# Attention and two gated layers on one core: output weights split earlier, transposes first, keys summed by two engines, another load order, two products in the drain

## The chip, the core and the metric

The kernel is one program on one core of a Trainium2 chip. TensorE multiplies and transposes into PSUM; VectorE (DVE), ScalarE (ACT) and GpSimd (POOL) work on what lies in SBUF, the first two on PSUM as well; SyncE (SP) issues every transfer between HBM and SBUF. Each engine runs its own list of instructions in order, and semaphores tie the lists together. The metric is the device time of one launch in microseconds (us). The kernel before took a median of 912.01 us over three runs, from 910.64 to 913.53.

## The reference

The input is attention with pooled keys and values, and two feed-forward layers behind it, all in float32:

```python
k_p = k.reshape(B, H, Sp, pool, D).mean(axis=3)          # B 4, H 8, S 576, D 64, pool 8
v_p = v.reshape(B, H, Sp, pool, D).mean(axis=3)          # Sp = 72
scores = scale * np.matmul(q, k_p.transpose(0, 1, 3, 2))
attn = softmax(scores)                                   # along the 72 keys
x = np.matmul(attn, v_p)                                 # then [2304 tokens, 512]
xn = x / rms(x) * rms_g                                  # layer 1: 512 -> 1536 -> 512
x = (silu(xn @ w_gate) * (xn @ w_val)) @ w_out
h = x @ w_in                                             # layer 2: 512 -> 2048 -> 512
out = silu(h) @ w_out2
```

`softmax` and `rms` stand for the written-out forms.

## The kernel before, in words

**Attention.** The 2304 tokens are 18 tiles of 128. For a batch element the 8 x 72 pooled rows of keys (values) are 576 rows of 512 numbers, loaded as five chunks of 128 rows (the last one has 64) into one of two `kv` slots. Summing eight neighbours is done for key batches 0 and 1 by DVE in one reduction per chunk group (`sum_keys`, L846), and otherwise by POOL in three halving additions (L505, L509, L513). DVE spreads the sums by masks into `kpm` (L855, keys) or `vb` (L871, values); TensorE transposes `kpm` (L1112) and ACT copies it to `kT` (L774).

A tile then goes through: transpose of q (L1122), scores (L1133), maximum and subtraction on DVE (`shift`, L881 and L886), exponential on ACT (L596), transpose of the weights (`prT`, L1144) and its copy on ACT (L779), the product with `vb` (L1161, "pv"), division on DVE (`divide`, L901 to L908), squares on ACT (L604), the reciprocal root on POOL (`ms` L564, `rstd` L569), its application on ACT (L609), transpose to features (L1174) and the scaled copy on DVE (L894). A hand-written list `order` sets how the steps of different tiles are interleaved; each engine walks the same list. Step s holds the scores of tile s, the `prT` of tile s-1, the q transpose of tile s+1, the x transpose of tile s-4 and the pv of tile s-1. While this runs, DVE makes the four sums of the first token block (`token_part` 0 to 3, L930 to L938) and its low halves (L942), from the x steps 6 to 14 on.

**Feed-forward.** The matrices are multiplied by a seven-product form of the 2 x 2 block product (`PRODUCTS`), in each of which a number is a high half plus a low half, with three matmuls per product of halves (L1227 to L1229). A unit is the seven products of 256 columns of an up-projection for 768 tokens: G (gate) and V (value) in layer 1. A "down" is the output projection that follows a pair of units (L1266 to L1268, 48 matmuls). Units run 0 (G), 1 (V), 2 (G), down 0, 3 (V), 4 (G), down 1 and so on.

**Weights.** Every raw weight block has to be loaded (`load_raw`), for a unit summed on POOL (`weight_sums`, L528 to L533, four instructions), rounded to high halves on ACT (`weight_high`, L629 to L634 or L622) and subtracted to low halves on POOL (`ring_low`, L540 to L546, four instructions, or `out_low`, L552 and L553 for an output block). POOL works through the list `made` in order: unit weights r0, r1, r2, output weights o0, r3, then r4, r5, o1 and on. r0 and the sums of r1 are made inside attention, between the `rstd` instructions; the rest begins when the last `rstd` is out. In ACT's list o0 stands behind the four high halves of the gated values (L704) of units 0 and 1, and r3 stands directly behind o0 and ahead of the silu of unit 2 (L686).

**Transfers.** SP issues all loads in one list: key and value batches, q tiles (`load_q(n)` waits until the q transpose of tile n-2 is done, since there are two buffers), raw weights. The loads of raw_a and raw_b (512 KB each) stand behind batch 1 of the keys, and batch 2 of keys and values stands behind q tile 4.

**First instructions.** POOL makes the identity and the masks; TensorE waits for all of them (`const_made`). DVE clears four pads and makes the mask tables, then waits for the first three chunks of keys.

Of the kernel before, what the change touches and what calls it, by code (L numbers as in the profile page):

```python
# [20 lines left out]
def ffn_kernel(nc, q, k, v, w_gate, w_val, w_out, rms_g, w2_in, w2_out, out):  # L21
# [13 lines left out]
    HB = H // 2  # L35
    H0 = [c * P // SP for c in range(RC)]
# [3 lines left out]
    FRONT = (3, 2)  # L40
# [32 lines left out]
    order = order[:order.index(("pv", NT - 1)) + 1] + [("x", NT - 3), ("unit", 0), ("x", NT - 1)]  # L73

# [58 lines left out]
    made = [("r", 0), ("r", 1), ("r", 2), ("o", 0), ("r", 3)]  # L133
# [64 lines left out]
    with ctx:  # L198
# [107 lines left out]
        s_const, s_kmask, s_pad = sem("const_made"), sem("kmask_made"), sem("pad_cleared")  # L306
# [3 lines left out]
        s_front = [sem("k0_front_loaded"), sem("v0_front_loaded")]  # L310
        s_frontsum = [sem("k0_front_summed"), sem("v0_front_summed")]
# [25 lines left out]
        def _(sp):  # L337
            def load_kv(b, kind):
                if b >= 2:
                    sp.wait_ge((s_ksum, s_vsum)[kind], b - 1)  # L340
                rows_v, done, dst = (k_rows, v_rows)[kind], (s_k, s_v)[kind][b % 2], KV[b % 2][kind]
                full, c0 = (RC - 1) * P, 0
                if b == 0:
                    c0 = FRONT[kind]
                    sp.dma_start(dst[:, 0:c0, :], rows_v[b, 0:c0 * P, :].rearrange("(c p) x -> p c x", p=P))\
                      .then_inc(s_front[kind], 16)
# [68 lines left out]
            load_q(0)  # L415
            load_kv(0, 1)
            load_q(1)
# [58 lines left out]
        def _(pool):  # L476
            level = [0]

            def step(ins):
# [7 lines left out]
            step(pool.affine_select(out=ident[:, :], in_=ident[:, :], compare_op=ALU.not_equal, fill=1.0,  # L487
                                    base=0, pattern=[[-1, P]], channel_multiplier=1))
# [71 lines left out]
            for n in range(NT):  # L560
# [9 lines left out]
                if n == 1:  # L570
                    weight_sums(0)
# [12 lines left out]
            ring_low(1)  # L584
            for i in range(2, len(made)):
# [7 lines left out]
        def _(act):  # L593
# [126 lines left out]
            def act_unit(x):  # L720
# [41 lines left out]
            for what, n in order:  # L762
# [20 lines left out]
                elif what == "pv":  # L783
# [38 lines left out]
        def _(dve):  # L822
            for i in range(2):
                for kind in range(2):
                    dve.memset(KV[i][kind][LAST:P, RC - 1, :], 0.0).then_inc(s_pad, 1)
            dve.wait_ge(s_const, 1)
            dve.tensor_scalar(vmask8[:, :, :], vmask[:, :, :], 1.0 / POOL, None, ALU.mult).then_inc(s_kmask, 1)
            for c in range(RC):
                e = H0[c] % 2
                dve.tensor_tensor(kmask[:, c, e:e + 1], vmask[:, c, 0:1], vmask[:, c, 2:3], ALU.add)\  # L830
                   .then_inc(s_kmask, 1)
                dve.tensor_copy(kmask[:, c, 1 - e:2 - e], vmask[:, c, 1:2]).then_inc(s_kmask, 1)
            for i in range(2):
                dve.tensor_copy(vb[i][:, :, :, D], vmask[:, :, :]).then_inc(s_kmask, 1)
            dve.wait_ge(s_kmask, 2 * RC + 3)
            dve.wait_ge(s_pad, 4)

            def sum_keys(b, part):
                lo, hi = (0, FRONT[0]) if part == 0 else (FRONT[0], RC)
                if b == 0 and part == 0:  # L840
                    dve.wait_ge(s_front[0], 16)
                else:
                    dve.wait_ge(s_k[b], 32)
                if b:
                    dve.wait_ge(s_kpm, b)
                ins = dve.tensor_reduce(kvp[:, 0, lo:hi, :],  # L846
                                        KV[b][0][:, lo:hi, :].rearrange("p c (r d) -> p c d r", r=POOL),
                                        AX.X, ALU.add)
                if part:
                    ins.then_inc(s_ksum, 1)  # L850
# [492 lines left out]
```

## Time and profile before

| what | us |
|---|---|
| median of three runs | 912.01 |
| the profiled execution, on its own | 909.02 |
| its span in the trace | 907.3 |
| TensorE busy in the span | 881.8 (97%) |
| TensorE busy, first 20 us | 8.62 |
| TensorE busy, 20 to 160 us | 129.2 of 140 |
| TensorE busy, 160 to 300 us | 140.00 of 140 |
| DVE busy | 519.0 (57%) |
| ACT busy | 341.4 (38%) |
| POOL busy | 252.2 (28%) |
| transfers | 191.67 MB, mean 211 GB/s |

The span runs from the first to the last instruction on the core; 909.02 is that same execution timed from outside, 1.7 us more, and 3.0 us under the median of the three plain runs. Busy time of TensorE is modelled from pipelined matmuls, so that a full slice need not be a slice at peak. Attention takes about the first 110 us, the feed-forward layers the rest.

### The profile page before, as it was taken

How to read it: one execution, taken by the hardware profiler on the slowest of the kernel's cores; microseconds unless marked ns; L12 is line 12 of the kernel's file. 1: busy time of each engine (PE TensorE's matmuls, PEld its weight loads, DVE VectorE, ACT ScalarE, POOL GpSimd, SP SyncE). 2: the span in 40 equal slices, each digit the busy share in tenths (PEclk: the TensorE clock that was granted, in tenths of full speed). 3: DMA queues.
4: the chain of work that ended last, by engine and by line, in shares of the span. 5: the costliest groups of instructions: out<-in, count | busy, mean ns of one | idle time of the engine just before them, and what ended most of it. 6: DMA issues, size and time to landing. Idle time of an engine off the chain costs nothing.

```text
span 907.3 us, 12808 instructions
## 1 busy us (share of the span) xinstructions
PE 881.8 (97%) x4902; PEld 831.6 (92%) x4902; DVE 519.0 (57%) x865; ACT 341.4 (38%) x668; POOL 252.2 (28%) x266
## 2 busy tenths in 40 slices
PE   4998998999999999999999999999999999999998
PEld 4887898999999999998989999999999898989897
DVE  7789863877655666666554445666554554343433
ACT  2566844444222232354554222322233332322322
POOL 2776378988200000637775000000000000000000
PEclk9999999999999999999999999999999999999999
DMA  9844256777875555257669666555544545475321
GB/s 273 224 126 122 104 203 236 280 279 278 336 283 204 209 209 209 79 223 277 244 255 390 240 233 248 204 205 204 207 183 181 201 174 209 174 277 175 128 90 73
DMA packets 55725, 191.67 MB, mean 211 GB/s; under 512 B 21872, under 2 KB 32112, under 8 KB 42608
## 3 DMA queue, kind: packets, MB, share of 16 engines
q1 hardware_dynamic: 55664, 190.85, 58.3%
q8 instruction: 39, 0.64, 0.3%
q14 instruction: 22, 0.18, 0.1%
HBM read 134.74 MB, written 56.10 MB: 210 GB/s over the span
## 4 chain that ended last, share of the span: by engine, by line
PE 85%; POOL 6%; issue 4%; DVE 2%; DMA 2%; ACT 1%; SPq 1%; POOLq 0%; ACTq 0%; DVEq 0%
PE ps L1227 15%; PE ps L1229 15%; PE ps L1228 15%; PE ps L1293 7%; PE ps L1294 7%; PE ps L1292 7%; PE ps L1268 5%; PE ps L1266 5%; PE ps L1267 5%; PE ps L1161 1%; PE ps L1133 1%; DMA qs<-in_q 1%; POOL wr L545 1%; POOL wr L546 1%; POOL rstd L569 1%
## 5 line engine op out<-in xcount | busy, mean ns | idle before, releaser
L1227 PE MATMUL ps<-xh,wr 128*128 128x384 f32 x840 | 281.8, 335 | 2.0 <-DVE qt L958 1.4
L1229 PE MATMUL ps<-xh,wr 128*128 128x384 f32 x840 | 281.2, 335 | 0.0
L1228 PE MATMUL ps<-xl,wr 128*128 128x384 f32 x840 | 280.9, 334 | 0.0
L1227 PEld LDWEIGHTS ps<-xh,wr 128*128 128x128 f32 x840 | 157.7, 188 | 4.5 <-DVE qt L958 3.0
L1228 PEld LDWEIGHTS ps<-xl,wr 128*128 128x128 f32 x840 | 157.7, 188 | 0.9
L1229 PEld LDWEIGHTS ps<-xh,wr 128*128 128x128 f32 x840 | 157.7, 188 | 0.0
L1294 PE MATMUL ps<-wo,al 128*128 128x512 f32 x288 | 112.5, 391 | 0.0
L1293 PE MATMUL ps<-wo,ah 128*128 128x512 f32 x288 | 112.4, 390 | 0.0
L1292 PE MATMUL ps<-wo,ah 128*128 128x512 f32 x288 | 112.0, 389 | 0.0
L1008 DVE TENSOR_TENSOR xacc<-ps,xacc 128x384 f32<-128x384 f32 (+1 forms) x102 | 62.5, 613 | 81.2 <-PE ps L1268 50.4
L1266 PE MATMUL ps<-ah,wo 128*128 128x384 f32 x288 | 97.2, 338 | 2.8 <-ACT qt L686 2.5
L704 ACT ACTIVATE ah<-qt 128x384 fp32r<-128x384 f32 x96 | 44.9, 517 | 139.2 <-PE ps L1294 126.2
L1268 PE MATMUL ps<-ah,wo 128*128 128x384 f32 x288 | 96.8, 336 | 0.0
L1267 PE MATMUL ps<-al,wo 128*128 128x384 f32 x288 | 96.8, 336 | 0.0
L995 DVE TENSOR_TENSOR al<-qt,ah 128x384 fp32r<-128x384 f32 x96 | 51.9, 583 | 73.3 <-ACT ah L704 73.3
L689 ACT ACTIVATE qt<-qt 128x384 f32<-128x384 f32 x126 | 65.5, 524 | 56.5 <-DVE qt L977 55.7
L977 DVE TENSOR_TENSOR qt<-ps,qt 128x384 f32<-128x384 f32 x84 | 46.2, 555 | 34.4 <-PE ps L1229 33.9
L1294 PEld LDWEIGHTS ps<-wo,al 128*128 128x128 f32 x288 | 54.0, 188 | 11.3
L1293 PEld LDWEIGHTS ps<-wo,ah 128*128 128x128 f32 x288 | 54.0, 188 | 10.8
L1292 PEld LDWEIGHTS ps<-wo,ah 128*128 128x128 f32 x288 | 54.1, 188 | 10.7
L704 ACT ACTIVATE ah<-vt 128x384 fp32r<-128x384 f32 x72 | 35.6, 520 | 66.3 <-DVE vt L988 66.3
L1266 PEld LDWEIGHTS ps<-ah,wo 128*128 128x128 f32 x288 | 54.6, 190 | 3.5 <-ACT qt L686 2.8
(128 smaller groups left out, 1152.6 us busy)
## 6 DMA issues: line engine op xcount, KB each, us to landing
wr<-ring_home SPq DMA_DIRECT2D x40, 1792.0 KB, 7.3
ring_home<-wr SPq DMA_DIRECT2D x20, 1792.0 KB, 8.1
wo<-out_home SPq DMA_DIRECT2D x28, 1024.0 KB, 4.8
out_home<-wo SPq DMA_DIRECT2D x14, 1024.0 KB, 9.5
raw_c<-in_moe_w_out SPq DMA_DIRECT2D x13, 512.0 KB, 7.1
qs<-in_q SPq DMA_DIRECT2D x16, 256.0 KB, 4.0
kv<-in_k SPq DMA_DIRECT2D x3, 1024.0 KB, 7.1
kv<-in_v SPq DMA_DIRECT2D x3, 1024.0 KB, 8.6
```

What stands on the lines that cost most here:

```text
L689: act.activation(qt[:, c, :], qt[:, c, :], ACT.Silu).then_inc(s_silu, 1)
L704: act.activation(ah[:, c, :], hidden(n)[:, c, :], ACT.Copy).then_inc(s_hi, 1)
L1008: dve.tensor_tensor(part, done, part, ALU.add).then_inc(s_rot, 1)
L1227: pe.matmul(out_ps, w_hi, x_hi, start=first and c == 0, stop=False, skip_group_check=True)
L1228: pe.matmul(out_ps, w_hi, x_lo, start=False, stop=False, skip_group_check=True)
L1229: ins = pe.matmul(out_ps, w_lo, x_hi, start=False, stop=c == 1, skip_group_check=True)
L1266: pe.matmul(out_ps, w_hi, h_hi, start=(rot or ends[0]) and c == 0, stop=False, skip_group_check=True)
L1267: pe.matmul(out_ps, w_hi, h_lo, start=False, stop=False, skip_group_check=True)
L1268: ins = pe.matmul(out_ps, w_lo, h_hi, start=False, stop=(rot or ends[1]) and c == 1, skip_group_check=True)
L1292: pe.matmul(out_ps, h_hi, w_hi, start=(rot or ends[0]) and c == 0, stop=False, skip_group_check=True)
L1293: pe.matmul(out_ps, h_hi, w_lo, start=False, stop=False, skip_group_check=True)
L1294: ins = pe.matmul(out_ps, h_lo, w_hi, start=False, stop=(rot or ends[1]) and c == 1, skip_group_check=True)
```

## The change

It has six parts.

1. **Start.** TensorE waits for the identity alone and runs 36 transposes of it into a PSUM bank that nobody reads (`WARM`). The mask tables and three of the four pads move from DVE to POOL. Key batch 0 is loaded as chunk 0, chunks 1 and 2, chunk 3 and the half chunk 4 (`KPARTS`); DVE sums chunks 0 to 3 in three reductions, POOL sums chunk 4.
2. **Load order.** q tile 1 goes ahead of value batch 0, key batch 2 ahead of q tile 4, and the two raw weight blocks behind q tile 5.
3. **Token sums.** `token_part` 0 to 3 move from x steps (6, 6, 7, 7) to (5, 6, 6, 8).
4. **Weights inside attention.** The sums of r0 move from POOL's n = 1 to n = 5, its low halves from 10 to 11; its high halves on ACT move one step later. The output block o0 stands second in `made`: high halves on ACT at pv 13, low halves on POOL at n = 14.
5. **Drain.** The first two products of unit 0 are issued ahead of pv 16 and pv 17.
6. **Waits.** The first unit of a phase waits for the low half of each product's operand, not for all seven.

```diff
-    FRONT = (3, 2)
+    KPARTS, VFRONT = [(0, 1), (1, 3), (3, RC - 1)], 2
+    for i in range(2):
+        order.insert(order.index(("pv", NT - 2 + i)), ("first", i))
-    made = [("r", 0), ("r", 1), ("r", 2), ("o", 0), ("r", 3)]
+    made = [("r", 0), ("o", 0), ("r", 1), ("r", 2), ("r", 3)]
...
             load_kv(0, 0)
             load_q(0)
+            load_q(1)
             load_kv(0, 1)
-            load_q(1)
             load_q(2)
             load_kv(1, 0)
...
-            load_raw(0)
-            load_raw(1)
             load_q(3)
             load_kv(1, 1)
+            load_kv(2, 0)
             for n in range(4, NT):
                 load_q(n)
-                if n in (4, 8):
-                    load_kv(n // 4 + 1, 0)
-                    load_kv(n // 4 + 1, 1)
+                if n == 4:
+                    load_kv(2, 1)
+                if n == 5:
+                    load_raw(made_at["r", 0])
+                    load_raw(made_at["r", 1])
...
-                if n == 1:
-                    weight_sums(0)
-                if n == 10:
+                if n == 5:
+                    weight_sums(0)
+                if n == 11:
                     ring_low(0)
                 if n == 12:
-                    weight_sums(1)
+                    weight_sums(made_at["r", 1])
+                if n == 14:
+                    out_low(made_at["o", 0])
...
-                    if n in (7, 8, 9):
-                        weight_high(0, (n - 7,))
+                    if n in (8, 9, 10):
+                        weight_high(0, (n - 8,))
+                    if n == 13:
+                        weight_high(made_at["o", 0])
...
-                    for i in {6: (0, 1), 7: (2, 3)}.get(n, (n - 4,) if 8 <= n < 15 else ()):
+                    for i in {5: (0,), 6: (1, 2), 7: (), 8: (3, 4)}.get(n, (n - 4,) if 9 <= n < 15 else ()):
...
-                if u == first_unit[ph]:
-                    pe.wait_ge(s_xlo, NF * (ph + 1))
-                for i, (bank, fw, fx, first) in enumerate(PRODUCTS):
+                for i, (bank, fw, fx, first) in list(enumerate(PRODUCTS))[begin:end]:
+                    if u == first_unit[ph]:
+                        pe.wait_ge(s_xlo, NF * ph + fx + 1)
...
-            pe.wait_ge(s_const, 1)
+            pe.wait_ge(s_ident, 1)
+            for _ in range(WARM):
+                pe.transpose(ps[:, 7, 0:P], ident[:, :], ident[:, :])
```

SP's list before, from the raw weights of the first units to the q tiles behind value batch 2:

```order
L370 DMA raw_a<-in_moe_w_gate 128x4x256
L370 DMA raw_b<-in_moe_w_val 128x4x256
L356 DMA qs<-in_q 128x8x64 [waits qT_made]
L347 DMA kv<-in_v 128x4x512
L349 DMA kv<-in_v 64x512
L356 DMA qs<-in_q 64x8x64 [waits qT_made]
L356 DMA qs<-in_q 64x8x64
L347 DMA kv<-in_k 128x4x512 [waits k_summed]
L349 DMA kv<-in_k 64x512
L347 DMA kv<-in_v 128x4x512 [waits v_summed]
L349 DMA kv<-in_v 64x512
L356 DMA qs<-in_q 128x8x64 [waits qT_made] x4
```

The same stretch of SP's list after the change; the two 64-row loads are q tile 4, and the q row behind value batch 2 is q tile 5:

```order
L365 DMA qs<-in_q 128x8x64 [waits qT_made]
L356 DMA kv<-in_v 128x4x512
L358 DMA kv<-in_v 64x512
L356 DMA kv<-in_k 128x4x512 [waits k0_part_summed,k_summed]
L358 DMA kv<-in_k 64x512
L365 DMA qs<-in_q 64x8x64 [waits qT_made]
L365 DMA qs<-in_q 64x8x64
L356 DMA kv<-in_v 128x4x512 [waits v0_front_summed,v_summed]
L358 DMA kv<-in_v 64x512
L365 DMA qs<-in_q 128x8x64 [waits qT_made]
L379 DMA raw_a<-in_moe_w_gate 128x4x256
L379 DMA raw_b<-in_moe_w_val 128x4x256
```

The raw weights left their place ahead of q tile 3 and stand behind q tile 5, and key batch 2 is ahead of q tile 4.

POOL's list before, at the end of r2 and the start of r3:

```order
L545 TENSOR_TENSOR wr<-wt,wr 128x512 [waits w_hi_made]
L546 TENSOR_TENSOR wr<-wt,wr 128x512
L552 TENSOR_TENSOR wo<-raw_f,wo 128x512 [waits w_hi_made]
L553 TENSOR_TENSOR wo<-raw_f,wo 128x512
L528 TENSOR_TENSOR wt<-raw_g 128x256 [waits w_raw_loaded6,ring_stored0,product_made]
```

The same place after the change:

```order
L572 TENSOR_TENSOR wr<-wt,wr 128x512 [waits w_hi_made]
L573 TENSOR_TENSOR wr<-wt,wr 128x512
L555 TENSOR_TENSOR wt<-raw_g 128x256 [waits w_raw_loaded6,ring_stored0,product_made]
L556 TENSOR_TENSOR wt<-raw_g 128x256
L558 TENSOR_TENSOR wt<-wt,raw_g 128x256 [waits w_sum_made]
```

The two instructions of o0 are gone from between r2 and r3; they stand between two `rstd` pairs inside attention.

TensorE's list after the change, from the x transpose of tile 14 into pv 17; before, the six matmul rows with `wr` were not there:

```order
L1191 MATMUL ps<-ident,xs 128x128 [waits xT_copied,xn_made]
L1191 MATMUL ps<-ident,xs 128x128 x3
L1244 MATMUL ps<-xh,wr 128x384 [waits shifted,x_lo_made,w_lo_made]
L1245 MATMUL ps<-xl,wr 128x384
L1246 MATMUL ps<-xh,wr 128x384
L1244 MATMUL ps<-xh,wr 128x384
L1245 MATMUL ps<-xl,wr 128x384
L1246 MATMUL ps<-xh,wr 128x384
L1178 MATMUL ps<-vb,prT 128x130 [waits x_made,v_blocks_made,prT_copied]
```

One product, six matmuls, stands between the transposes of a tile and the pv that waits for ACT's copy.

## Rows read from the trace of the kernel before

**Rows 1.** Stretches: length, busy us and count of each engine, clock, DMA.
```profile
0.00:20.00 20.00, 8.62 (x34) 7.34 (x35) 13.56 (x26) 3.81 (x5) 5.66 (x22) 1.00 0.95 268
120.00:140.00 20.00, 17.09 (x95) 16.13 (x94) 12.08 (x19) 7.61 (x14) 13.11 (x14) 1.00 0.75 283
140.00:150.00 10.00, 9.74 (x47) 9.74 (x48) 2.20 (x4) 3.82 (x8) 9.12 (x11) 0.83 0.44 185
...
160.00:300.00 140.00, 140.00 (x807) 139.71 (x806) 91.09 (x148) 51.27 (x96) 65.01 (x58) 1.00 0.73 281
```

**Rows 2.** Timeline of the start: start, us, engine, what, [idle before].
```profile
12.01 1.81 POOL L505 TENSOR_TENSOR kv<-kv 128x768 f32<-128x768 f32 x1 [8.79 <-DMA kv<-in_v]
12.99 2.26 PE L1133 MATMUL ps<-kT,qT 128*128 128x144 f32 x8 [0.83 <-ACT kT L774]
...
14.98 0.59 POOL L513 TENSOR_TENSOR kvp<-kv 128x192 f32<-128x192 f32 x1
...
16.76 1.15 DVE L871 TENSOR_TENSOR vb<-kvp,vmask 128x960 f32<-128x960 f32 x1
...
19.28 0.76 DVE L881 TENSOR_REDUCE mx<-ps 128x8 f32<-128x576 f32 x1 [1.38 <-PE ps L1133]
...
27.58 1.25 PE L1133 MATMUL ps<-kT,qT 128*128 128x144 f32 x8
...
29.21 0.60 PE L1122 MATMUL ps<-ident,qs 128*128 128x128 f32 x4
...
35.70 0.66 PE L1122 MATMUL ps<-ident,qs 128*128 128x128 f32 x4 [0.34 <-DMA qs<-in_q]
```

**Rows 3.** The chain that ended last, 20 to 40 us: start, us, what.
```profile
23.11 0.52 SPq L349
...
26.00 9.65 DMA qs<-in_q
```

**Rows 4.** Transfers issued from 23.1 to 23.6 us: size, us to landing.
```profile
kv<-in_k SPq DMA_DIRECT2D x1, 128.0 KB, 8.0
```

**Rows 5.** Timeline of the middle of attention, DVE, TensorE and POOL.
```profile
74.47 0.94 DVE L935 TENSOR_TENSOR xt<-xacc,xt 128x768 f32<-128x768 f32 x1
...
77.59 1.93 PE L1161 MATMUL ps<-vb,prT 128*128 128x130 f32 x12 [1.28 <-DVE xs L908]
...
80.98 1.71 PE L1133 MATMUL ps<-kT,qT 128*64 128x144 f32 x16 [1.46 <-issue]
...
84.91 2.09 DVE L942 TENSOR_TENSOR xl<-xacc,xh 128x768 fp32r<-128x768 f32 x1
...
86.13 2.00 POOL L546 TENSOR_TENSOR wr<-wt,wr 128x512 fp32r<-128x512 f32 x1
```

**Rows 6.** Timeline from the drain to unit 4, all engines.
```profile
104.17 1.97 PE L1161 MATMUL ps<-vb,prT 128*128 128x130 f32 x12 [0.41 <-ACT prT L780]
...
108.04 1.96 PE L1161 MATMUL ps<-vb,prT 128*128 128x130 f32 x12 [0.77 <-ACT prT L780]
...
113.66 1.28 POOL L540 TENSOR_TENSOR wr<-raw_b,wr 128x512 fp32r<-128x512 f32 x1
...
118.53 0.42 PE L1227 MATMUL ps<-xh,wr 128*128 128x384 f32 x1
...
126.40 0.44 PE L1227 MATMUL ps<-xh,wr 128*128 128x384 f32 x1 [0.33 <-POOL wr L546]
...
131.47 1.29 POOL L552 TENSOR_TENSOR wo<-raw_f,wo 128x512 fp32r<-128x512 f32 x1 [5.13 <-ACT wo L622]
...
137.95 0.63 ACT L629 ACTIVATE wr<-raw_g 128x512 fp32r<-128x512 f32 x1 [6.55 <-POOL wt L533]
...
140.26 0.69 PE L1266 MATMUL ps<-ah,wo 128*128 128x384 f32 x1 [2.46 <-ACT qt L686]
...
143.62 0.37 PE L1267 MATMUL ps<-al,wo 128*128 128x384 f32 x1
...
159.15 0.44 PE L1227 MATMUL ps<-xh,wr 128*128 128x384 f32 x1 [1.44 <-DVE qt L958]
```

More of the change, by code:

```diff
@@ L35, in ffn_kernel @@
     HB = H // 2
+    WARM = 36
     H0 = [c * P // SP for c in range(RC)]
@@ L309, in ffn_kernel @@
         s_v = [sem(f"v_loaded{i}") for i in range(2)]
-        s_front = [sem("k0_front_loaded"), sem("v0_front_loaded")]
-        s_frontsum = [sem("k0_front_summed"), sem("v0_front_summed")]
+        s_kpart = [sem(f"k0_part_loaded{i}") for i in range(2)]
+        s_vfront, s_kpartsum, s_vfrontsum = sem("v0_front_loaded"), sem("k0_part_summed"), sem("v0_front_summed")
         s_kpmfront = sem("k0_front_masked")
@@ L486, in _ @@
             step(pool.memset(vmask[:, :, :], 1.0))
-            step(pool.affine_select(out=ident[:, :], in_=ident[:, :], compare_op=ALU.not_equal, fill=1.0,
-                                    base=0, pattern=[[-1, P]], channel_multiplier=1))
+            pool.affine_select(out=ident[:, :], in_=ident[:, :], compare_op=ALU.not_equal, fill=1.0,
+                               base=0, pattern=[[-1, P]], channel_multiplier=1).then_inc(s_ident, 1)
             for c in range(RC):
@@ L499, in _ @@
             last.then_inc(s_const, 1)
+            pool.wait_ge(s_const, 1)
+            pool.tensor_scalar(vmask8[:, :, :], vmask[:, :, :], 1.0 / POOL, None, ALU.mult).then_inc(s_kmask, 1)
+            for c in range(RC):
+                e = H0[c] % 2
+                pool.tensor_tensor(kmask[:, c, e:e + 1], vmask[:, c, 0:1], vmask[:, c, 2:3], ALU.add)\
+                    .then_inc(s_kmask, 1)
+                pool.tensor_copy(kmask[:, c, 1 - e:2 - e], vmask[:, c, 1:2]).then_inc(s_kmask, 1)
+            for i in range(2):
+                pool.tensor_copy(vb[i][:, :, :, D], vmask[:, :, :]).then_inc(s_kmask, 1)
+            pool.wait_ge(s_kmask, 2 * RC + 3)
+            for i, kind in ((0, 1), (1, 0), (1, 1)):
+                pool.memset(KV[i][kind][LAST:P, RC - 1, :], 0.0).then_inc(s_pad, 1)
             def pool_pairs(b, kind, lo, hi):
                 t, n = KV[b % 2][kind], POOL * D // 2
-                pool.wait_ge(s_pad, 4)
+                pool.wait_ge(s_pad, 3)
+                if (b, kind) == (0, 0):
+                    pool.wait_ge(s_pad0, 1)
                 pool.wait_ge((s_k, s_v)[kind][b % 2], 32 * (b // 2 + 1))
@@ L578, in _ @@
                             pool_rest(b, kind, 0)
-                if n == 10:
+                if n == 5:
+                    weight_sums(0)
+                if n == 11:
                     ring_low(0)
                 if n == 12:
-                    weight_sums(1)
-            ring_low(1)
-            for i in range(2, len(made)):
+                    weight_sums(made_at["r", 1])
+                if n == 14:
+                    out_low(made_at["o", 0])
+            ring_low(made_at["r", 1])
+            for i in range(3, len(made)):
                 if made[i][0] == "r":
@@ L822, in _, with sum_keys @@
         def _(dve):
[L823 to L850, printed above, removed]
-                elif b == 0:
-                    ins.then_inc(s_frontsum[0], 1)
+            def sum_keys(b, lo, hi):
+                return dve.tensor_reduce(kvp[:, 0, lo:hi, :],
+                                         KV[b][0][:, lo:hi, :].rearrange("p c (r d) -> p c d r", r=POOL),
+                                         AX.X, ALU.add)
             def mask_keys(lo, hi):
@@ L1311, in _ @@
                     transpose_x(n)
+                elif what == "first":
+                    unit(0, n, n + 1)
                 elif what == "unit":
-                    unit(n)
+                    unit(n, 2)
             for kind, x in items[1:]:
```

77 lines of the change are left out of this document (48 added, 29 removed).

## The prediction

> **What bounds the kernel now.** I read the stretches first. From 160 to 300 us TensorE is busy 140.00 of 140 us [rows 1]: there is nothing to win there but work, and the change removes none. The first 20 us have 8.62 busy, 120 to 140 us have 17.09, and in 140 to 150 us the granted clock is 0.83 [rows 1]. So the gain can only lie in pauses of TensorE ahead of 160 us, and whatever TensorE gains there reaches the end undiminished. The waits of TensorE, read as rows of the timeline, then give four places: the start, where q tile 5 is waited for although every engine ahead of it is slow too [rows 2, 3]; steps 11 and 12, where DVE is late [rows 5]; the drain, where two pv wait for ACT [rows 6]; and the opening of the feed-forward part, where r2, o0 and r3 follow one another on POOL [rows 6].
>
> **1. The start: 1.5 us.** Two things limit it, the transfers and DVE.
>
> Transfers. In the order of before, the second piece of key batch 2 lands at 23.11 + 8.0 = 31.1 us [rows 3, 4] and q tile 5 at 26.00 + 9.65 = 35.65 [rows 3]. Between them lie value batch 2 and one q tile, 1.44 MB in 4.55 us, 316 GB/s. The raw blocks of 1.05 MB that leave are then 3.3 us. After the change the transfers up to key batch 2 and q tile 4 are those of before less the raws, so q tile 4 lands at 31.1 - 3.3 = 27.8, and q tile 5 at 32.4.
>
> DVE. The key sums start on smaller chunks and without tables ahead of them, so I expect kT some 2 us earlier. But value batch 0 now stands behind q tile 1 (0.26 MB, estimated 1 us by 0.26 / 316 GB/s = 0.83 and one more issue), so POOL, which began its sum at 12.01 when the values had come [rows 2], begins at 13.0. It needs 3.56 us (14.98 + 0.59 - 12.01), so `vb` on DVE starts at 16.6 where it started at 16.76, and takes 1.15 [rows 2]. In DVE's list the second `shift` stands behind `vb`: it begins at 17.8. Before it waited for slow scores and began at 19.28 [rows 2]. That is 1.5 us, and DVE has no pause of note between there and 31 us, so everything follows 1.5 us earlier. The q transpose of tile 4, at 29.21 [rows 2], is wanted at 27.7 and its data are there at 27.8: 0.1 to 0.3 lost. Tile 5 was wanted 0.34 ahead of 35.70 [rows 2]; wanted now at 34.1, landed at 32.4. So 35.70 becomes 34.1 or so. I take 1.5. The bounds: 0.3 if only the wait for q tile 5 goes and DVE gains nothing; 3.3 if the transfer alone decided.
>
> The warm-up transposes: eight score matmuls took 2.26 us at 12.99 and 1.25 at 27.58, while the column of the granted clock reads 1.00 for the whole stretch [rows 1, 2]; by the durations the first ran at half the speed, the 1.2 GHz level, after an engine that had stood still. The transposes may bring the full speed forward, worth 1 us on the first scores; but the second `shift` waits for `vb`, which hangs on the values, so I cost it at nothing. They have ended, at 36 x 0.15 to 0.22 us from 1.6, by 7 to 9.6 us, before the first `kpm` comes, so they cost nothing either; at worst they hold the first key transposes by 0.6.
>
> The mask tables and three pads on POOL (15 small instructions and three clears) end around 8 us; chunk 4 then takes 1 to 1.5 us. If that is 1 us late, `kT` is late by that much, but still ahead of `vb`. Nothing.
>
> **2. The middle: 2.2 us.** At x step 7 DVE made two token sums of 0.94 us each (L935, L938; one is shown) [rows 5] right behind the masks of key batch 3; then came the division for which TensorE waited 1.28 us, and the late `shift` led through ACT to 1.46 us in front of the scores at 80.98 [rows 5]. Without the 1.9 us DVE is that much earlier, and TensorE's two pauses of 2.74 shrink to about 1: 1.8 gained. The sum that moves to step 5 goes into a pause of DVE that waits for pv; the one in step 8 goes where DVE waited for the scores. Further, the low halves of r0 moved from POOL's n = 10 to 11: the L942 of 2.09 us, which lay under L546 of 2.00 [rows 5], is 1 us without it, but now `vb` of batch 3 lies beside them. I give 0.4 for both. Bounds: 3.7 if all pauses of that stretch go; -1.0 if the added sum and the collisions land in front of a pv.
>
> Here the shared port speaks against the change. The row: beside L546 on POOL, both with two inputs from SBUF, L942 takes 2.09 and L546 2.00, where their like take 0.94 (L935, as wide) and 1.28 (L540) [rows 5, 6]. The Trainium skill (SBUF — State Buffer, section "SBUF: two separate sides") says that DVE with two SBUF inputs and GpSimd share one port pair as an exclusive lock, and the loser blocks for the whole instruction. By that rule the trace agrees, and every piece put on POOL beside DVE can cost a blocked instruction on either side; at one of 1.28 us in front of `vb` of batch 3 the sum of this part would be 0.9 instead of 2.2.
>
> ACT gets o0's high halves at pv 13 (1.04 us by their like in `weight_high`) in a step of 4.5 us in which it had a pause: 0. POOL gets sums at n = 5 (2.9 us) and o0's lows at n = 14 (2.9 us). It waits over 2 us for the squares before most `ms`, and the result is used a step later: 0.
>
> **3. The drain and unit 1: 0.8 us.** Product 0 (six matmuls 0.174 apart, 1.04 us) goes ahead of the pv at 104.17 and product 1 ahead of that at 108.04; the pauses there are 0.41 and 0.77 by modelled ends, 0.57 and 0.96 by issue [rows 6]. So 2.08 us of work fill 1.53 of pause and delay pv 17 by 0.5. ACT copied product 0 ahead of the last squares and no longer waits for it (0.7 us), so the last `rstd` comes 0.4 earlier and r1's lows start at 113.2 for 113.66 [rows 6]. They take 4.5 (three of 1.28, one of 0.7), so unit 1 starts at 117.75 for 118.53; unit 0 ends at 117.0, and 0.75 us are a new wait of TensorE for POOL.
>
> **4. The opening of the feed-forward part: 5.7 us more.** From the start of r1's lows to unit 2 it is 12.7 us before (113.66 to 126.40) and that chain stays, so unit 2 starts at 126.0, after a wait of 0.9. Here the gain is down to 0.4. It ends 7.5 us later, at 133.5, and down 0 starts at once, for 134.38 before, as o0 is long made: 0.85. Then the big piece. Before, POOL stood 5.13 us for o0's high halves at 131.47, did the lows in 2.85, then r3's sums; ACT therefore waited 6.55 us at 137.95, and the silu of unit 2 behind it held TensorE for 2.46 at 140.26 [rows 6]. In this stretch the clock fell to 0.83 in the mean [rows 1]: ten matmuls from 140.26 to 143.62 took 3.36 us for 1.74 [rows 6]. Now POOL goes from r2 straight to r3's sums (126.0 to 128.9), ACT rounds them behind the four L704, at 130.0 to 132.1, the silu's product is ready at 131.2, and down 0 wants it at 136.6. So 2.6 of pause and 1.6 of slow clock go: down 0 ends at 141.9 for 147.0, a gain of 5.1. r3 is ready at 135.4, r4 at 143.5, r5 at 151.6, o1 at 154.7, against unit 3 at 141.9, unit 4 at 149.2 and down 1 at 156.5: each ahead of its use, since a group of two units and a down takes TensorE 23 us and POOL 19.5. Before, ACT waited in the same way for r5 and ended in 1.44 us at 159.15 [rows 6]; that goes too. Total from the drain on 6.5. Bounds: 3.0 if only o0's wait and half the silu's stall go; 7.4 if the new waits at units 1 and 2 do not come.
>
> **Sum.** 1.5 + 2.2 + 0.8 + 5.7 = 10.2 us. The profiled execution, 909.02 (span 907.3 and 1.7 around it), becomes 898.8; it stands 3.0 under the median, so the median of 912.01 becomes 901.8.
>
> **Rivals.**
> - *The start and the middle give nothing; the opening does.* The values of batch 0 come later, DVE's list waits for them, and the sums moved in attention collide. For it: 316 GB/s of transfers are full from the start [rows 1, 3]. Against it: 3.3 us of raws leave that queue, and 1.9 us of DVE work leave the place that waits. Only 6.5 remain: 905.5.
> - *The wait moves to r1 and r2.* POOL's last `rstd` hangs on pv 17, which the two products delay; if that costs 1 us and ACT is again behind at r3, the opening gives 3.0, and the total is 6.7 or less: 905.5 too. Against it: POOL's idle of 5.13 us is in front of o0 alone.
> - *Everything comes out better:* 3.3 + 3.7 + 7.4 = 14.4, 897.6, if the early path is bound by transfers only and the port is quiet.
> - *Slower, at 915.* POOL becomes the bound inside attention. The sums at n = 5 (2.9), r0's lows at 11 (4.5) and o0's lows at 14 (2.9) delay `rstd`, and that the normalisation and the x transposes; it decides from the point where POOL's pause before `ms` and the step of slack behind it are both used up. If all 10.3 us reached TensorE, at three pauses with the clock falling each time by 1.6 as at 140.26, 15.1 us would be lost against 10.2 won: +4.9 on 912.0, with some overlap 915. Against it: r0's sums and lows stood on POOL before and TensorE did not wait for `rstd` in any row.
> - *The change does not do what it says:* ACT, not POOL, holds r3, since its list is in order; then down 0 waits as before and the kernel is within 2.5 us, 909.5, by the start alone.
>
> **How the numbers follow.** Forecast 0.62, with an own range of 899 to 904.5; first rival 0.13, second 0.10, better 0.08, slower 0.03, not as it says 0.04. The predicted time is 901.8; the range for 8 in 10 is 897 to 906.5. Up to 2.7 us (0.3%) either way is what a measurement of this kernel can hardly tell from no change: faster 0.93, within 0.04, slower 0.03.
>
> **What would show it.** Right: q tile 5 transposed near 34 us and not waited for; the second `shift` behind `vb` near 17.8; no pause over 1 us in front of pv 11; unit 1 and unit 2 each after a short wait for POOL; no pause in down 0 and a clock of 1.00 from 130 to 160 us; all 140 us busy after unit 3. Wrong: a wait for q tile 4 of over 1 us, a `vb` later than 18 us, a TensorE wait for `rstd` or the normalised tile in attention, or a unit between 3 and 8 that waits for its weights.

## The result, and the profile after

| | before | after |
|---|---|---|
| median of 4 runs each | 911.4 us (910.64 to 913.53) | 901.49 us (899.81 to 903.01) |
| profiled execution, its span | 909.02, 907.3 us | 899.81, 898.1 us |

The ratio is 0.9887, 95% interval [0.9862, 0.9913]: 9.9 us by the medians, 9.2 us by the profiled spans. The forecast of 901.8 us stands. But one of its four terms is almost wholly missing, and another is a good deal larger than worked out. The four runs after lie 3.2 us apart, and the mean granted clock goes with them: 1.00 in the fastest, 0.992 in the slowest.

I read where the 9.2 us were gained by setting the same instruction of TensorE side by side in both traces. What counts is how far the gain has grown at each:

| TensorE reaches | before | after | gain so far |
|---|---|---|---|
| q tile 4 | 29.21 | 27.12 | 2.09 |
| pv 4 | 41.06 | 38.52 | 2.54 |
| pv 8 | 61.34 | 58.80 | 2.54 |
| pv 9 | 65.87 | 65.52 | 0.35 |
| pv 13 | 89.25 | 86.54 | 2.71 |
| pv 15 | 99.64 | 96.95 | 2.69 |
| unit 1 | 118.53 | 115.08 | 3.45 |
| unit 2 | 126.40 | 123.26 | 3.14 |
| down 0 | 134.38 | 130.69 | 3.69 |
| end of the span | 907.3 | 898.1 | 9.2 |

The stretches first, as in [rows 1]: length, busy us and count of TensorE, its weight loads, DVE, ACT and POOL, granted clock, DMA share, GB/s.
```profile
0.00:20.00 20.00, 14.35 (x89) 12.83 (x90) 12.48 (x13) 5.73 (x9) 10.71 (x41) 1.00 1.01 270
120.00:140.00 20.00, 19.41 (x112) 19.09 (x111) 13.10 (x21) 7.82 (x15) 17.47 (x19) 1.00 0.56 238
...
140.00:150.00 10.00, 10.00 (x59) 9.77 (x58) 6.43 (x11) 4.94 (x9) 9.12 (x10) 1.00 0.63 236
...
160.00:300.00 140.00, 140.00 (x807) 139.64 (x806) 88.05 (x146) 48.50 (x91) 56.33 (x51) 1.00 0.71 272
```
From 120 to 140 us TensorE is busy 19.41 us for 17.09, and the clock of 0.83 from 140 to 150 us is 1.00 now [rows 1]. The same stretch from 160 us on is as full as before. The 14.35 of the first 20 us mislead: 6.64 of them are the 36 warm-up transposes.

The start in the timeline of after (start, us, engine, what, idle before), for [rows 2]:
```profile
11.07 1.22 PE L1150 MATMUL ps<-kT,qT 128*128 128x144 f32 x8 [0.83 <-ACT kT L803]
12.86 1.81 POOL L532 TENSOR_TENSOR kv<-kv 128x768 f32<-128x768 f32 x1 [3.73 <-DMA kv<-in_v]
...
16.44 1.16 DVE L876 TENSOR_TENSOR vb<-kvp,vmask 128x960 f32<-128x960 f32 x1 [2.56 <-POOL kvp L540]
17.52 0.75 DVE L886 TENSOR_REDUCE mx<-ps 128x8 f32<-128x576 f32 x1
...
27.11 0.81 DVE L860 TENSOR_TENSOR kpm<-kvp,kmask 128x640 f32<-128x640 f32 x1
27.12 0.66 PE L1139 MATMUL ps<-ident,qs 128*128 128x128 f32 x4 [0.49 <-DMA qs<-in_q]
...
32.99 0.60 PE L1139 MATMUL ps<-ident,qs 128*128 128x128 f32 x4
```
POOL begins the value sum when its data land, `vb` follows, and the second `shift` stands right behind `vb` on DVE at 17.52, for 19.28 before [rows 2]. Tile 5 of q waits for nothing; tile 4 now does, by 0.49.

Behind it `kpm` of batch 1 is shorter too, 0.81 for 1.21. In the timeline of before it began beside POOL's pairs, which ended at 29.39; after, POOL's pairs ended at 25.57, ahead of it:
```profile
26.33 3.06 POOL L505 TENSOR_TENSOR kv<-kv 128x512 f32<-128x512 f32 x2 [10.76 <-DMA kv<-in_v]
...
28.87 1.21 DVE L855 TENSOR_TENSOR kpm<-kvp,kmask 128x640 f32<-128x640 f32 x1
```

The middle in the timeline of after, for [rows 5]:
```profile
58.35 3.06 POOL L532 TENSOR_TENSOR kv<-kv 128x512 f32<-128x512 f32 x2
59.63 2.58 DVE L935 TENSOR_TENSOR xt<-xacc 128x768 f32<-128x768 f32 x1
...
62.87 1.54 POOL L536 TENSOR_TENSOR kv<-kv 128x640 f32<-128x640 f32 x1
63.17 2.25 DVE L876 TENSOR_TENSOR vb<-kvp,vmask 128x960 f32<-128x960 f32 x1
65.52 1.94 PE L1178 MATMUL ps<-vb,prT 128*128 128x130 f32 x12 [2.16 <-DVE vb L876]
...
69.86 3.04 POOL L532 TENSOR_TENSOR kv<-kv 128x512 f32<-128x512 f32 x2
...
71.62 1.96 DVE L860 TENSOR_TENSOR kpm<-kvp,kmask 128x640 f32<-128x640 f32 x1
...
76.07 0.83 PE L1129 MATMUL ps<-ident,kpm 128*128 128x128 f32 x5 [1.12 <-issue]
```
This is new. The token sum that the change moved to step 5 takes 2.58 us beside POOL's pairs, and ends 0.8 us behind them; `vb` of batch 2 is then late and, beside POOL's next sum, takes 2.25 us for 1.15; TensorE stands for 2.16 us in front of pv 9. All of the lead of 2.54 us but 0.35 is gone here, and comes back by pv 13, since the waits of before at pv 11 and the scores behind it [rows 5] are smaller.

From the drain to unit 3, for [rows 6]:
```profile
101.98 1.86 PE L1178 MATMUL ps<-vb,prT 128*128 128x130 f32 x12
...
110.02 0.55 POOL L598 TENSOR_TENSOR rstd<-ms,half 128x1 f32<-128x1 f32 x1
110.53 1.29 POOL L567 TENSOR_TENSOR wr<-raw_b,wr 128x512 fp32r<-128x512 f32 x1
...
123.26 0.45 PE L1244 MATMUL ps<-xh,wr 128*128 128x384 f32 x1 [0.59 <-POOL wr L573]
...
127.30 0.61 ACT L660 ACTIVATE wr<-raw_g 128x512 fp32r<-128x512 f32 x1
...
129.09 0.46 ACT L717 ACTIVATE qt<-ps 128x384 f32<-128x384 f32 x1
...
130.69 0.33 PE L1283 MATMUL ps<-ah,wo 128*128 128x384 f32 x1
...
139.01 0.34 PE L1244 MATMUL ps<-xh,wr 128*128 128x384 f32 x1
```
ACT rounds r3 at 127.30, for 137.95 after an idle time of 6.55 [rows 6]; the silu behind it runs at 129.09, well ahead of its use. Down 0 goes through in 8.32 us (130.69 to 139.01), for 12.75 before (134.38 to 147.13) with its stop of 2.46 and slow matmuls [rows 6].

### The profile page after: what moved, and what is told of

It reads as the page before. It is cut to its first block, busy times and chain, and to the rows that moved or that the text cites. A ratio compares the mean times of both kernels' runs of the same rounds, so it can differ in the third digit from the quotient of the medians.

```text
span 898.1 us, 12923 instructions
## 1 busy us (share of the span) xinstructions
PE 882.7 (98%) x4938; PEld 833.0 (93%) x4938; DVE 518.7 (58%) x850; ACT 341.7 (38%) x668; POOL 257.7 (29%) x285
## 4 chain that ended last, share of the span: by engine, by line
PE 88%; POOL 4%; issue 3%; DVE 3%; SPq 1%; DMA 1%; ACT 0%; POOLq 0%; DVEq 0%; ACTq 0%
PE ps L1244 16%; PE ps L1246 15%; PE ps L1245 15%; PE ps L1310 7%; PE ps L1311 7%; PE ps L1309 7%; PE ps L1285 6%; PE ps L1283 6%; PE ps L1284 6%; PE ps L1178 1%; PE ps L1150 1%; DMA kv<-in_v 1%; POOL rstd L598 1%; DVE kvp L855 1%; POOL wr L572 0%
```

## Experiments

Each kernel is the changed one with the edit shown. Step by step comparisons are of profiled runs; the starts differ by up to 4 us at tile 5 of q between runs (experiment 5, which loses 8.9, set aside), from when tile 4 lands and from stretches of slow clock; so each stage is measured from an instruction at its own beginning: the middle from pv 8 to pv 13, the drain and the opening from pv 15. In that measure before has 27.91 and 26.76 us (pv 15 to unit 2), after 27.74 and 26.31.

**1. o0 back behind r2.** Its high halves, lows and place in the list as before; all the rest as changed.
```diff
-    made = [("r", 0), ("o", 0), ("r", 1), ("r", 2), ("r", 3)]
+    made = [("r", 0), ("r", 1), ("r", 2), ("o", 0), ("r", 3)]
-    EARLY = {("o", 0): 4, ("r", 2): 5, ("r", 3): 6}
+    EARLY = {("r", 2): 4, ("o", 0): 5, ("r", 3): 6}
```


> The changed kernel with one part undone: o0 is fourth in the list again, its high halves on ScalarE stand behind the gated values of unit 1 and its low halves on GpSimd between r2 and r3. Theory A (the opening of the feed-forward part is bound by the chain r2, o0, r3 on GpSimd and ScalarE): the wait for o0 of about 0.4 us at down 0, the pause of about 2.5 us for the silu of unit 2 with the slow clock behind it (1.6 us) and the 1.4 us in unit 4 all come back; 5.5 to 6.5 us slower than the changed kernel, near 907.5. Rival B (the gain there came from attention ending earlier, which let GpSimd start the chain earlier; the place of o0 matters little): under 2 us slower.

Measured: 908.6 us median of 10 (906.52 to 913.12), ratio to before 0.9975 [0.9953, 0.9996]; span 905.1. The medians are 7.1 us apart; the spans, 7.0, of which 0.8 arise ahead of pv 15. The waits of before are back, in its timeline:
```profile
131.96 0.45 PE L1281 MATMUL ps<-ah,wo 128*128 128x384 f32 x1 [0.37 <-POOL wo L580]
...
135.54 0.63 ACT L658 ACTIVATE wr<-raw_g 128x512 fp32r<-128x512 f32 x1 [6.56 <-POOL wt L560]
...
137.85 0.44 PE L1281 MATMUL ps<-ah,wo 128*128 128x384 f32 x1 [2.48 <-ACT qt L715]
...
156.74 0.45 PE L1242 MATMUL ps<-xh,wr 128*128 128x384 f32 x1 [1.38 <-DVE qt L961]
```
Unit 2 stands 26.26 us behind pv 15, as in after; from unit 2 to the end it is 781.10 us (905.1 - 124.00) for 774.84 after (898.1 - 123.26) and 780.9 before. So 6.3 us hang on this one edit, within the expected 5.5 to 6.5: some two thirds of the gain. It is shown.

**2. Token sums at the old steps.**
```diff
-  for i in {5: (0,), 6: (1, 2), 7: (), 8: (3, 4)}.get(n, (n - 4,) if 9 <= n < 15 else ()):
+  for i in {6: (0, 1), 7: (2, 3)}.get(n, (n - 4,) if 8 <= n < 15 else ()):
```


> The changed kernel with the four token sums back at x steps 6, 6, 7, 7. Theory A (the first sum at step 9 lay beside the first additions of key batch 3 on GpSimd, 2.58 us instead of 0.95, and the value blocks beside the second, 2.25 instead of 1.15, so pv 9 waited 2.16 us): the wait at pv 9 goes, L935 for the first sum is at most 1.2 us; in exchange the pauses in front of pv 11 and the scores of tile 13 come back, about 2.7 us; between pv 8 and pv 13 the distance stays 27.5 to 28.2 us (27.7 in the changed kernel, 27.9 before). Rival B (the value blocks of batch 2 are late because GpSimd does the sums of r0 at n = 5 ahead of them): pv 9 still waits about 2 us and the distance grows to about 30 us.

Measured: 900.21 us, one run. Pv 8 to pv 13 takes 27.41 us, for 27.74 with the move and 27.91 before; pv 9 waits for nothing, and the first sum takes 1.19. The scores behind pv 11 wait 1.46 again. So the move costs 0.33 us, where I had counted 1.8 gained. (27.41 lies just under the 27.5 of theory A.)

**3. No warm-up transposes.**
```diff
-    WARM = 36
+    WARM = 0
```


> The changed kernel without the 36 transposes at the start. Theory A (the second shift waits for the value blocks, so the speed of TensorE ahead of it is hidden): the scores of tile 0 take about 2.3 us instead of 1.22, the second shift still starts at 17.5 to 17.8 us and q tile 5 is transposed at 33.0 to 33.3; no loss beyond 0.5 us. Rival B (TensorE at half speed is on the path): second shift and q tile 5 later by 1 to 2 us, the span 1 to 2 us longer.

Measured: 901.43 us, one run. The first scores take 2.26 us again (at 11.11), and the first pv starts at 17.70 for 17.75: they bring nothing at the start, as costed. But the span is 899.7, 1.6 longer than after's, where I had expected no loss beyond 0.5. It stands in the middle of its timeline, and in its stretches:
```profile
65.44 3.05 PE L1178 MATMUL ps<-vb,prT 128*128 128x130 f32 x12 [2.15 <-DVE vb L876]
68.41 2.29 PE L1150 MATMUL ps<-kT,qT 128*128 128x144 f32 x8
```
```profile
60.00:70.00 10.00, 7.85 (x43) 6.77 (x43) 9.83 (x13) 4.92 (x12) 6.90 (x8) 0.80 0.64 180
70.00:80.00 10.00, 9.98 (x66) 8.97 (x65) 8.40 (x13) 8.10 (x16) 6.58 (x6) 0.86 0.30 74
```
Here the same wait at pv 9 is followed by a granted clock of 0.80 and 0.86, and scores of 2.29 us for 1.25, the 1.2 GHz level. Pv 8 to pv 13 takes 29.26 (58.72 to 87.98) for 27.74. Seven profiles have this wait. In four (after, experiments 4, 6 and 10) the clock stays 1.00 in that stretch; in three it falls: to 0.86 in experiment 1 and 0.83 in experiment 5, which have the warm-up, and here. What decides it I could not settle, nor whether the missing warm-up has a part in it; the new wait cost from nothing to 1.5 us above its length, from run to run.

**4. The two products back behind the pv.**
```diff
-    for i in range(2):
-        order.insert(order.index(("pv", NT - 2 + i)), ("first", i))
-                    unit(n, 2)
+                    unit(n)
```


> The changed kernel without the two early products: all seven products of unit 0 stand behind pv 17 and the x transpose of tile 15. Theory A (1.5 us of pauses of TensorE are filled, but units 1 and 2 wait for GpSimd's low halves, so only 0.5 to 1 us arrives): unit 1 starts 1 to 1.6 us later than at 115.08 counted from pv 15, unit 2 0.3 to 0.9 us later than its 26.3 us behind pv 15. Rival B (all filled time arrives): unit 2 starts 1.5 to 2 us later counted from pv 15.

Measured: 900.67 us, one run. In its timeline the pauses of before are back, and the wait for POOL at unit 2 is smaller:
```profile
101.83 1.96 PE L1176 MATMUL ps<-vb,prT 128*128 128x130 f32 x12 [0.40 <-ACT prT L807]
105.71 1.96 PE L1176 MATMUL ps<-vb,prT 128*128 128x130 f32 x12 [0.78 <-ACT prT L807]
...
124.06 0.44 PE L1242 MATMUL ps<-xh,wr 128*128 128x384 f32 x1 [0.30 <-POOL wr L571]
```
Unit 1 starts 18.92 us behind pv 15 for 18.13, unit 2 26.76 for 26.31. The products are worth 0.79 at unit 1, less than the 1 to 1.6 that I had expected, and 0.45 where it counts, at unit 2. POOL's chain takes the rest: its last `rstd` ends at 111.35 here, 14.05 behind pv 15, and at 110.57 in after, 13.62 behind.

**5. The raw blocks back ahead of q tile 3,** all other loads in the new order.
```diff
+            load_raw(made_at["r", 0])
+            load_raw(made_at["r", 1])
             load_q(3)
```


> The changed kernel with the two raw weight loads (1.05 MB) back ahead of q tile 3; the rest of the load order stays changed. Theory A (the start is bound by transfers, and moving the raws is what frees it): q tile 4 lands about 3.3 us later, its transpose moves from 27.1 to about 30.4, q tile 5 from 33.0 to about 35.5 and the span grows by 2.5 us. Rival B (the start is bound by VectorE behind the value blocks): q tile 4 is transposed by 28 us and the span grows by less than 1 us.

Measured: 908.51 us, one run, with one of before beside it at 910.29. Its timeline, and its stretch from 20 to 40 us:
```profile
32.43 1.11 PE L1138 MATMUL ps<-ident,qs 128*128 128x128 f32 x4 [5.49 <-DMA qs<-in_q]
...
34.62 3.58 PE L1177 MATMUL ps<-vb,prT 128*128 128x130 f32 x12
38.14 3.20 PE L1149 MATMUL ps<-kT,qT 128*64 128x144 f32 x16
```
```profile
20.00:40.00 20.00, 13.62 (x76) 11.51 (x76) 10.53 (x16) 6.52 (x15) 7.54 (x8) 0.78 0.95 235
```
The place of the loss is as expected, its size is not: tile 5 of q is reached at 41.87, 8.9 us later than in after, where I had expected 2.5. Of these 5.3 are tile 4 (32.43 for 27.12; 3.3 are the 1.05 MB at 316 GB/s, the other 2.0 are open) and 3.6 come behind it: 9.44 us from tile 4 to tile 5 for 5.87. After a pause of 5.49 us the clock is 0.78 in the mean of the stretch, and twelve matmuls of a pv take 3.58 us for 1.96. With key batch 2 ahead of tile 4, the start works only if the raws leave this place; what moving the raws alone was worth, in the order of before, this run does not say.

**6. Key batch 2 behind q tile 4.**
```diff
-            load_kv(2, 0)
             for n in range(4, NT):
                 load_q(n)
                 if n == 4:
+                    load_kv(2, 0)
```


> The changed kernel with key batch 2 behind q tile 4 instead of ahead of it. Theory A (q tile 4 waits for the 3.9 us transfer of key batch 2, DVE is right behind it): no wait for q tile 4, its transpose at 26.6 to 26.9 where it is 27.1, q tile 5 then waits for its own data or not, at 32.4 to 33.0: between 0 and 0.6 us better. Rival B (the wait for q tile 4 is the bound of the start): 1.3 us or more better at q tile 5.

Measured: 901.48 us, one run: no gain. Tile 4 no longer waits (27.33), but tile 5 is reached at 34.67, later than in either expectation, and the key transposes behind tile 4 start at 29.48 for 28.07. The delay begins ahead of the loads moved, of which the first is issued at 16.98 in after:
```profile
15.11 2.26 PE L1150 MATMUL ps<-kT,qT 128*128 128x144 f32 x8 [0.88 <-DVE pr L891]
...
27.12 1.54 POOL L536 TENSOR_TENSOR kv<-kv 128x640 f32<-128x640 f32 x1
...
27.70 1.64 DVE L860 TENSOR_TENSOR kpm<-kvp,kmask 128x640 f32<-128x640 f32 x1
```
In this run the second scores took 2.26 us for 1.22 in spite of the warm-up (the granted clock is 0.66 from 10 to 20 us), DVE was 0.6 late, and `kpm` fell beside POOL's L536, which itself had begun 1.5 us later: 1.64 us for 0.81. 0.6 + 0.8 are the 1.4. What the order of these two loads is worth stays open.

**7. Token sums at x steps 6, 6, 8, 8:** none in step 5, none in step 7. The third 8 in the edit is the first low half, which stands there in every version.
```diff
-  for i in {5: (0,), 6: (1, 2), 7: (), 8: (3, 4)}.get(n, (n - 4,) if 9 <= n < 15 else ()):
+  for i in {6: (0, 1), 7: (), 8: (2, 3, 4)}.get(n, (n - 4,) if 9 <= n < 15 else ()):
```


> The changed kernel with the token sums at x steps 6, 6, 8, 8 in place of 5, 6, 6, 8: none stands at steps 9 or 11. Theory A (each VectorE instruction with two SBUF inputs beside a GpSimd addition waits for it; the first sum at step 9 caused the 2.16 us at pv 9, and a third instruction in step 12 fits into slack): no wait over 0.4 us at pv 9, and pv 8 to pv 13 is 25.5 to 26.5 us (27.7 in the changed kernel, 27.4 with the old places). Rival B (VectorE is simply full here, and every place costs the same): the distance stays 27.2 to 28 us.

Measured: 901.6 us, one run with a late start: tile 4 of q was waited for by 1.95, and behind that wait the clock fell (0.66 from 30 to 40 us), so that tile 5 was reached at 37.14. From pv 8 to pv 13 it takes 25.66 us, for 27.74 in after. In its timeline:
```profile
28.58 0.66 PE L1139 MATMUL ps<-ident,qs 128*128 128x128 f32 x4 [1.95 <-DMA qs<-in_q]
29.81 3.44 PE L1178 MATMUL ps<-vb,prT 128*128 128x130 f32 x12
...
66.00 1.15 DVE L876 TENSOR_TENSOR vb<-kvp,vmask 128x960 f32<-128x960 f32 x1
...
69.13 1.19 DVE L935 TENSOR_TENSOR xt<-xacc 128x768 f32<-128x768 f32 x1
...
73.59 1.96 DVE L860 TENSOR_TENSOR kpm<-kvp,kmask 128x640 f32<-128x640 f32 x1
```
`vb` takes 1.15 us and pv 9 waits for nothing. Beside experiment 2 this splits the move in two: taking the pair out of step 7 is worth 27.41 - 25.66 = 1.75 us, and putting one sum into step 5 (with one more from 8 to 6) costs 27.74 - 25.66 = 2.08.

**8 and 9. As 7, and POOL's value sums of batch 3 one step later,** so that `kpm` of batch 3 has no work of POOL beside it. One run, then six.
```diff
-                        if n == 4 * b - 6 + 2 * kind:
+                        late = b == 3 and kind == 1
+                        if n == 4 * b - 6 + 2 * kind + late:
```


> The kernel with the token sums at 6, 6, 8, 8 and with GpSimd's sums of value batch 3 one step later (its first additions at n = 9, the rest at n = 10). Theory A (the mask product of key batch 3, 1.96 us at 71.6 instead of 0.8 to 1.2, was blocked by those additions): L860 of key batch 3 takes at most 1.3 us and pv 8 to pv 13 shrinks by a further 0.5 to 1.2 us against the kernel with the token sums alone. Rival B (the length of that product has another cause, or the additions block something else as much): no change beyond 0.3 us.

> The version with the token sums at steps 6, 6, 8, 8 and GpSimd's value sums of batch 3 one step later, now timed. If the 1.7 us that its single profile lay below the changed kernel's (span 896.4 against 898.1) are the middle's (25.88 us from product 8 to product 13 against 27.74), the median comes out about 899.5 to 900, ratio to the kernel before 0.9865 to 0.988, that is 1.5 to 2 us below the changed kernel in the same job. Rival: the later starts wander by as much (the fourth late query tile was transposed between 27.1 and 28.6 us in the runs so far), and the two medians lie within 0.8 us of each other.

Measured: 898.16 us in the one run; 898.52 median of 6 (898.26 to 903.17), ratio 0.9872 [0.9844, 0.9901]. The timeline of the timed one:
```profile
62.16 1.15 DVE L877 TENSOR_TENSOR vb<-kvp,vmask 128x960 f32<-128x960 f32 x1
62.57 2.14 POOL L536 TENSOR_TENSOR kv<-kv 128x640 f32<-128x640 f32 x1
...
69.75 0.81 DVE L861 TENSOR_TENSOR kpm<-kvp,kmask 128x640 f32<-128x640 f32 x1
...
73.38 3.76 POOL L532 TENSOR_TENSOR kv<-kv 128x512 f32<-128x512 f32 x2
...
75.50 2.46 DVE L944 TENSOR_TENSOR xt<-xacc,xt 128x768 f32<-128x768 f32 x1
```
`kpm` falls from 1.96 to 0.81 us with nothing else altered in it: the stretching is POOL's doing. But the pairs now meet a token sum, 2.46 us for 0.95, and pv 8 to pv 13 takes 25.88 in both profiles: 0.2 longer than in 7, where I had expected 0.5 to 1.2 less. The first two rows show the same pair as in after's middle, the other way round: here `vb` began first and keeps its 1.15 us, and POOL's L536, 0.4 us behind it, takes 2.14 for 1.54; there POOL began first, by 0.3, and `vb` took 2.25.

**10. The changed kernel again,** timed beside 9 as its base.


> The changed kernel itself, timed beside the one above as its base: median 901 to 902, ratio 0.9885 to 0.9895; its profile shows the 2.58 us first token sum beside GpSimd's key pairs again, and product 8 to product 13 in 27.5 to 28 us.

Measured: 900.37 median of 6 (899.75 to 903.32), ratio 0.9883 [0.9859, 0.9907]; span 898.2; pv 8 to pv 13 27.71 us. Both medians are lower than I expected, their distance is as expected: version 9 is 1.85 us lower. The intervals of the ratios overlap. Compare runs whose mean granted clock reads 1.00: version 9's four took 898.26 to 898.55, the changed kernel's three 899.75 to 900.09, 1.5 us apart; and the 1.8 us of the middle in the profiles say where it comes from. Version 9 is the fastest of those timed more than once. By the middle alone version 7 is as good, so POOL's later step is not shown to add anything to it.

**11. Token sums at the old steps, POOL's value sums of batch 3 one step later.**


> The token sums back where the kernel before has them (two at step 6, two at step 7), with GpSimd's value sums of batch 3 one step later. Theory (VectorE's operations stretch only while GpSimd's pairs run): the key mask of batch 3 takes 0.82 us instead of 1.96, and all four sums about 0.95 to 1.2 us, since none lies beside the pairs; product 8 to product 13 takes 26.2 to 26.8 us (27.41 with the old places alone, less 1.14). Rival (VectorE's queue is full there whatever the pairs do): 27.2 or more.

Measured: 899.39 us, one run. Pv 8 to pv 13 26.26 us, within the theory's 26.2 to 26.8 and below the rival's 27.2. In its timeline:
```profile
70.35 0.81 DVE L861 TENSOR_TENSOR kpm<-kvp,kmask 128x640 f32<-128x640 f32 x1
...
71.68 0.95 DVE L941 TENSOR_TENSOR xt<-xacc,xt 128x768 f32<-128x768 f32 x1
72.66 0.96 DVE L944 TENSOR_TENSOR xt<-xacc,xt 128x768 f32<-128x768 f32 x1
```
It differs from experiment 2 in POOL's one step alone, and is shorter by 1.15 us (27.41 to 26.26): exactly what `kpm` lost by being blocked (1.96 to 0.81).

## Why the prediction was right, and where it was not

The mechanism was right in the part that carries most of the gain, and the total was right with the help of two errors of opposite sign. That the median came so close (901.49 for 901.8) is luck besides: the profiled execution came at 899.81 for 898.8, and the median lies 1.7 above it, where I had added before's 3.0.

| term | predicted | measured | from |
|---|---|---|---|
| 1. start | 1.5 | 2.54 | pv 4 |
| 2. middle | 2.2 | 0.15 | 2.69 at pv 15 less 2.54 |
| 3. drain and unit 1 | 0.8 | 0.76 | 3.45 at unit 1 less 2.69 |
| 4. opening | 5.7 | 5.75 | 9.2 less 3.45 |
| sum | 10.2 | 9.2 | |

*The start, undersized by 1.0.* The chain was the one named: values at 12.86 (I had 13.0), `vb` at 16.44 (16.6), second `shift` at 17.52 (17.8), which is 1.76 earlier, not 1.5. I had then let DVE's list run at its old pace. It ran faster: `kpm` of batch 1 took 0.81 for 1.21 (27.11 after, 28.87 before), 0.4 more, and the wait of 0.34 at tile 5 [rows 2] is gone, which I had counted among the causes but not added. 1.76 + 0.40 + 0.34 = 2.50. The 0.4 is POOL's doing as well: its pairs no longer run beside this `kpm`. Keys came earlier as foreseen (`kT` at 10.28 for 12.20); which part of the new start bought it, the small chunks, the tables on POOL or the order of the loads, no run separates. The transfer of tile 4 was predicted for 27.8 and came at 27.1. Nothing came of the warm-ups, as costed, and experiment 3 shows it. The rival in which start and middle give nothing was refuted by the start alone.

*The middle, oversized by 2.05: the term that failed.* The step was: "The sum that moves to step 5 goes into a pause of DVE that waits for pv". It did go there (DVE would have waited for 1.2 us, as in experiment 7), but I had looked only at DVE's row. In the same pause POOL does the pairs of key batch 3, which POOL's own list places right behind `rstd` of step 6, and both have two inputs in SBUF. The 0.95 us became 2.58, its end moved `vb` beside POOL's next sum (2.25 for 1.15), and pv 9 waited 2.16. The other half of the step held: "1.8 gained" by clearing step 7 is 1.75 by experiments 2 and 7. Together 1.75 - 2.08, and 0.5 from elsewhere (27.91 before to 27.41 in experiment 2). That is the 0.4 that I had given for r0's lows: the L942 of 2.09 us [rows 5] takes 0.95 at its place in after, and the pause of 0.46 in front of pv 13, which TensorE had before, is gone. So the mechanism that I weighed as speaking against the change, the port shared by DVE and GpSimd, was right, and I had put it to a wrong place: r0's lows beside `vb` of batch 3, at a price of 1.28. There it cost nothing: `vb` takes 1.15 at 85.06, and the lows begin at 86.86. The Trainium skill (SBUF — State Buffer, section "SBUF: two separate sides") calls it an exclusive lock for the whole instruction; the trace agrees: 2.58 is the rest of POOL's pairs (58.35 + 3.06 - 59.63 = 1.78) and then nearly the whole sum. My lower bound of the part (-1.0) held it.

*The drain, right.* R1's lows start 3.13 us earlier (110.53 for 113.66), 2.69 of them the lead at pv 15: 0.44, where I had said 0.4. They take 4.5, unit 1 follows (the wait of 0.75 that I had put in front of it is hardly there, 0.1 by the modelled end of the transposes at 115.00; one of 0.27 stands inside unit 0, at 109.64), and unit 2 is 0.45 better by experiment 4 and by before (26.76 to 26.31). The rival of waits moved to r1 and r2 was half there (0.59 at unit 2, as forecast near 0.9) and cost no more, since r3 was in time. What part 6 of the change, the waits for single operands, is worth was not measured.

*The opening, right.* From unit 2 to the end I had 6.5 - 0.4 = 6.1; it is 6.06 (780.90 to 774.84), and undoing this edit alone costs 6.26 (experiment 1). At first it was 6.50: in unit 4 DVE's first sum stands at 148.91 for 158.55, a lead of 9.64 for 3.14 at unit 2. By 858.06 (867.27 before) the lead is 9.21. So my "whatever TensorE gains there reaches the end undiminished" held but for 0.4 us, and no run shows where these go. Its three pieces are seen singly: no wait in front of down 0, no stop and no slow clock in it (8.32 us for 12.75), no 1.44 at unit 4 [rows 6]. The rival in which ACT holds r3 was refuted by its row at 127.30.

*Slower, at 915,* had POOL as the bound of attention. POOL did cost 2.08 there, but by blocking DVE, not by a late `rstd`; TensorE's waits in attention name DVE, ACT, a transfer or issue, and POOL only for the identity at the start.

## What to carry to other kernels

When an operation moves into a pause, read the row of the engine that shares its port in the same microseconds, not only its own: a token sum put into a free 1.2 us of VectorE cost 2.08 us, since two-input work ran on GpSimd beside it; in the next step it cost nothing. Raise the order of a producer (here the output weights' halves) ahead of the first engine that stands idle for it; an in-order list turned one late operand into three waits and a slow clock, 6 us in all. And measure a change in a stage from an instruction at the stage's own beginning, or the start's scatter of some us hides effects of 1 to 2.

## What the runs showed of the hardware

- DVE's operations with two inputs in SBUF, alone and beside POOL's: `kpm` 128x640 0.81 and 1.96; token sum 128x768 0.95 and 2.46 to 2.58; `vb` 128x960 1.15 and 2.25. The one that begins second is the one that takes longer, in the rows of after's middle and of experiment 9: POOL's L536 is 1.54 when ahead of `vb` and 2.14 when behind it. Before's middle fits: L942 at 84.91, with POOL's L545 just begun (84.90), took 2.09, and POOL's L546, which came while L942 ran, 2.00 [rows 5]. So a shift of 0.4 us decides which engine pays, and it matters only where that engine is waited for. The Trainium skill (SBUF — State Buffer, section "Who interferes with whom") has it so: "Issue order, not op shape, decides who blocks."
- The granted clock reads 1.00 for before's first 20 us, while eight score matmuls take 2.26 us; in experiment 6 the record has 0.66 from 10 to 20 us and the same 2.26. By durations both ran at the 1.2 GHz level for a while, so in the first microseconds durations are the better witness.
- Waits of TensorE of one length do not end alike. One of 2.12 to 2.16 us in front of pv 9 was followed by full speed in four profiles and by a mean clock of 0.80 to 0.86 over ten us in three. One of 1.67 and one of 1.76 us for tile 4 (experiments 2 and 11) left the clock at 1.00, one of 1.95 (experiment 7) was followed by 0.66 over ten us, one of 5.49 (experiment 5) by 0.78 in the mean of 20 to 40 us.
